# Softmax reciprocals brought to 64 partitions through HBM, and value products in four bursts per pair of heads

## The reference

```python
scores = scale * np.matmul(q, k.transpose(0, 1, 3, 2))
thresh = np.max(scores, axis=-1, keepdims=True) - tau
scores = np.where(scores >= thresh, scores, -1000000000.0)
attn = np.exp(scores - np.max(scores, axis=-1, keepdims=True))
attn = attn / (np.sum(attn, axis=-1, keepdims=True) + 1e-09)
x = np.matmul(attn, v)                      # then (tokens, heads * dim)
h = x @ moe_w_in;  x = (h * np.tanh(softplus(h))) @ moe_w_out
h = x @ moe2_w_in; out = (h * np.clip(h + 3, 0, 6) / 6) @ moe2_w_out
```

## Time and profile before

| | us |
|---|---|
| median of three runs | 1125.66 |
| the profiled execution | 1125.93 |
| its span | 1124.2 |
| PE, busy share of the span | 1108.1 (99%) |
| ACT | 489.7 (44%) |
| DVE | 423.8 (38%) |
| POOL | 263.5 (23%) |

### The profile page before, as it was taken

One profiled execution on the slowest core, in us unless ns is written; L12 is line 12 of the kernel. 1 busy time (PEld: TensorE's weight loads), 2 busy tenths in 40 slices (PEclk: granted clock), 3 DMA queues, 4 the chain that ended last, 5 costly groups with the idle time before them and its releaser, 6 DMA issues.

```text
span 1124.2 us, 15233 instructions
## 1 busy us (share of the span) xinstructions
PE 1108.1 (99%) x6064; PEld 880.3 (78%) x6064; DVE 423.8 (38%) x903; ACT 489.7 (44%) x882; POOL 263.5 (23%) x179
## 2 busy tenths in 40 slices
PE   6999999999999999999999999999999999999998
PEld 5767676767668888889888888888888888888887
DVE  7888787888822111112121111123223223222222
ACT  6777787778744232223222233442232232232232
POOL 6677558655622200000000015420000000000000
PEclk9999999999999999999999999999999999999999
DMA  7432223222021000000000022300010010010010
GB/s 223 127 107 65 84 64 106 64 70 80 12 103 47 1 1 1 1 1 1 1 1 1 19 94 75 112 2 1 1 38 1 1 38 0 1 38 1 1 39 20
DMA packets 42488, 46.09 MB, mean 41 GB/s; under 512 B 3504, under 2 KB 30128, under 8 KB 42416
## 3 DMA queue, kind: packets, MB, share of 16 engines
q1 hardware_dynamic: 42416, 45.10, 13.4%
HBM read 40.37 MB, written 4.72 MB: 40 GB/s over the span
## 4 chain that ended last, share of the span: by engine, by line
PE 97%; DVE 1%; ACT 1%; issue 1%; DMA 0%; SPq 0%; DVEq 0%; ACTq 0%
PE banks L486 35%; PE banks L459 12%; PE banks L461 12%; PE banks L460 12%; PE banks L406 8%; PE banks L353 7%; PE banks L365 5%; PE banks L361 3%; PE banks L386 2%; DVE probs L706 0%; DVE neg_max L722 0%; ACT exps L569 0%; DMA k_raw<-kT 0%; ACT probsT L534 0%; DVE totals L738 0%
## 5 line engine op out<-in xcount | busy, mean ns | idle before, releaser
L767 DVE SCALAR_TENSOR_TENSOR g_low<-gate,g_high 128x512 fp32r<-128x512 f32 (+1 forms) x160 | 102.8, 643 | 478.2 <-ACT g_high L642 478.2
L459 PE MATMUL banks<-x_low,w_in_high 128*128 128x512 f32 (+1 forms) x640 | 239.4, 374 | 0.0
L461 PE MATMUL banks<-x_high,w_in_high 128*128 128x512 f32 (+1 forms) x640 | 238.8, 373 | 0.0
L460 PE MATMUL banks<-x_high,w_in_low 128*128 128x512 f32 (+1 forms) x640 | 237.2, 371 | 0.0
L642 ACT ACTIVATE g_high<-gate 128x512 fp32r<-128x512 f32 (+1 forms) x160 | 94.4, 590 | 310.4 <-PE banks L486 309.9
L459 PEld LDWEIGHTS banks<-x_low,w_in_high 128*128 128x128 f32 x640 | 120.5, 188 | 23.3 <-issue 0.6
L461 PEld LDWEIGHTS banks<-x_high,w_in_high 128*128 128x128 f32 x640 | 120.0, 187 | 23.5
L460 PEld LDWEIGHTS banks<-x_high,w_in_low 128*128 128x128 f32 x640 | 120.7, 189 | 22.4
L722 DVE TENSOR_REDUCE neg_max<-banks 128x1 f32<-128x576 f32 x144 | 108.8, 756 | 50.2 <-PE banks L353 49.9
L486 PE MATMUL banks<-g_low,w_out_high 128*128 128x512 f32 (+1 forms) x320 | 118.3, 370 | 0.8 <-issue 0.8
L486 PE MATMUL banks<-g_high,w_out_low 128*128 128x512 f32 (+1 forms) x320 | 117.8, 368 | 0.0
(11 more groups left out here) (59 smaller groups left out, 1429.8 us busy)
## 6 DMA issues: line engine op xcount, KB each, us to landing
q_raw<-qT SPq DMA_DIRECT2D x64, 144.0 KB, 2.8
k_raw<-kT SPq DMA_DIRECT2D x64, 144.0 KB, 2.8
w_in_raw<-w_in SPq DMA_DIRECT2D x16, 512.0 KB, 4.2
w_out_raw<-w_out SPq DMA_DIRECT2D x16, 512.0 KB, 4.6
out<-x SPq DMA_DIRECT2D x18, 256.0 KB, 2.9
values<-v SPq DMA_DIRECT2D x16, 256.0 KB, 3.1
values<-v SPq DMA_DIRECT2D x16, 32.0 KB, 2.8
tau_in<-tau SPq DMA_DIRECT2D x1, 0.5 KB, 2.8
```

Source lines behind the costliest of these rows:

```text
L459: nc.tensor.matmul(bank, w_in_high[:, t, cols], low, start=(t == 0), stop=False)
L460: nc.tensor.matmul(bank, w_in_low[:, t, cols], high, start=False, stop=False)
L461: mm = nc.tensor.matmul(bank, w_in_high[:, t, cols], high, start=False, stop=(t == KT - 1))
L767: nc.vector.scalar_tensor_tensor(out=g_low[:, f % 2, 0:width], in0=gate[:, f % 2, 0:width], scalar=1 / 6 if layer_of(c) else 1.0, in1=f32( ...
```

## The change

`spread_sums` and ACT's copy of it are dropped. The nine reciprocal columns are instead turned to nine rows by one TensorE transpose in step 2 (`turn_recips`, between the tail transpose and the main ones), into spare columns of a score buffer. ACT copies the rows to SBUF (`keep_recips`), issues a transfer of them to HBM (`store_recips`, 4.6 KB), and in step 4 issues three transfers that read them back, repeated on 64 partitions, to `spread` (`load_spread`). Each head's row lies in one piece or, for the second head, in two. The store waits for the copy, the loads for the store, `scale_mixed` for the loads. Score tile 3, which uses the same buffer, waits for the copy.

The value products of a pair, spread over seven steps before, run in four bursts: part 0 in steps 4 (two key tiles) and 6 (three), part 1 in steps 0 and 1 of the next set (two, three). `scale_mixed` moves from steps 6 and 1 to 8 and 3. In the join the products of each part run in one burst, `turn` is written out, and the wait for `x` stands ahead of the first `down`.

```diff
+    recip_rows = place("recip_rows", [PAIR_TILES, P])
...
+    recip_dram = nc.dram_tensor("recip_dram", (2, PAIR_TILES * P), F32, kind="Internal").ap()
...
+        turned_recips = [banks[0:PAIR_TILES, 2 * s, BANK - P:BANK] for s in range(3)]
...
+        def recip_slot(pair):
+            return 0 if pair < PAIRS - 1 else 2
...
                 if g == EARLY_PIECES:
                     sp.wait_ge(x_ready, 2 * PAIRS)
-                    sp.wait_ge(spread_kept, 2 * PAIRS)
...
+                    if half == 0 and i == 3:
+                        after(pe, recip_rows_kept, t // PAIR_TILES)
...
-            def turn(t, s):
+            def turn_tail(t, s):
                 pe.wait_ge(probs_ready, t + 1)
                 nc.tensor.transpose(turned_tail[s % 3], probs[:, s % 3, SEQ - P:SEQ], ident[:, :]).then_inc(tail_turned, 1)
+            def turn_main(t, s):
                 after(pe, main_kept, t)
                 for j in range(MAIN):
                     mm = nc.tensor.transpose(turned[:, P * j:P * j + P], probs[:, s % 3, P * j:P * j + P], ident[:, :])
                 mm.then_inc(main_turned, 1)
-            def spread_sums(pair, b, u):
-                if u == 0:
-                    pe.wait_ge(recips_ready, pair + 1)
+            def turn_recips(pair, b):
+                pe.wait_ge(recips_ready, pair + 1)
+                nc.tensor.transpose(turned_recips[recip_slot(pair)], recips[:, b, :], ident[:, :]).then_inc(recips_turned, 1)
+            def mix(it, pair, b, u, keys):
+                if keys[0] == 0 and u == 0:
+                    pe.wait_ge(v_loaded[b], 32 * (it + 1 if b == 0 else it))
                     after(pe, x_ready, 2 * pair)
-                else:
-                    pe.wait_ge(spread_kept, 2 * pair + 1)
-                for i in range(MAIN + 1):
-                    c0, c1 = max(P * i, PART_AT[u]), min(P * i + P, PART_AT[u + 1])
-                    for a in range(2):
-                        if c0 < c1:
-                            full = i < MAIN
-                            rows = slice(0, P) if full else slice(TAIL * a, TAIL * a + TAIL)
-                            col = a * (MAIN + 1) + i if full else MAIN
-                            first = 0 if full else TAIL * a
-                            mm = nc.tensor.matmul(mixed[u][DH * a:DH * a + DH, c0 - PART_AT[u]:c1 - PART_AT[u]],
-                                                  recips[rows, b, col:col + 1].to_broadcast([rows.stop - rows.start, DH]),
-                                                  ident[rows, first + c0 - P * i:first + c1 - P * i], start=True, stop=True)
-                mm.then_inc(spread_ready, 1)
-            def mix(it, pair, b, u, keys):
-                if keys[0] == 0 and u == 0:
-                    pe.wait_ge(v_loaded[b], 32 * (it + 1 if b == 0 else it))
-                    pe.wait_ge(spread_kept, 2 * pair + 2)
                     pe.wait_ge(main_kept, (pair + 1) * PAIR_TILES)
                     pe.wait_ge(tail_kept, (pair + 1) * PAIR_TILES)
                 if keys[0] == 0 and u == 1:
@@ -410,8 +407,8 @@
-            part0 = {4: (0,), 5: (1, 2), 6: (3, 4)}
-            part1 = {7: (0, 1), 8: (2,), 0: (3,), 1: (4,)}
+            part0 = {4: (0, 1), 6: (2, 3, 4)}
+            part1 = {0: (0, 1), 1: (2, 3, 4)}
...
             def attention_step(it, s, ahead=True):
@@ -421,16 +418,15 @@
                     score_tile(it, s)
                 pair, b = it * PAIRS_IT + p - 1, (p + 1) % 2
                 if not first or p == 1:
-                    if i in (2, 3):
-                        spread_sums(pair, b, i - 2)
                     if i in part0:
                         mix(it, pair, b, 0, part0[i])
-                    if i in (7, 8):
-                        mix(it, pair, b, 1, part1[i])
-                if not first and i in (0, 1):
+                if not first and i in part1:
                     mix(it, pair - 1, 1 - b, 1, part1[i])
                 if (not first or s >= 2) and (ahead or s < 2):
-                    turn(t - 2, (s - 2) % TILES_IT)
+                    turn_tail(t - 2, (s - 2) % TILES_IT)
+                    if i == 2 and (not first or p == 1):
+                        turn_recips(pair, b)
+                    turn_main(t - 2, (s - 2) % TILES_IT)
...
-            ups_early = {0: 0, 1: 1, 3: 2, 7: 3}
+            UPS_EARLY = 4
...
-            for s in range(PAIR_TILES + 2):
-                if s in ups_early:
-                    pe.wait_ge(tail_kept, ITS * TILES_IT - 2 + ups_early[s] // 2)
-                    up(0, ups_early[s])
-                attention_step(ITS, s, ahead=False)
-            pe.wait_ge(tail_kept, ITS * TILES_IT)
+            def up_early(f):
+                pe.wait_ge(tail_kept, ITS * TILES_IT - 2 + f // 2)
+                up(0, f)
+            last_pair, last_b = PAIRS - 1, PAIRS_IT - 1
+            up_early(0)
+            mix(ITS, last_pair - 1, 1 - last_b, 1, range(MAIN + 1))
+            turn_tail(ITS * TILES_IT - 2, TILES_IT - 2)
+            turn_main(ITS * TILES_IT - 2, TILES_IT - 2)
+            turn_tail(ITS * TILES_IT - 1, TILES_IT - 1)
+            turn_main(ITS * TILES_IT - 1, TILES_IT - 1)
+            turn_recips(last_pair, last_b)
+            up_early(1)
+            up_early(2)
+            mix(ITS, last_pair, last_b, 0, range(MAIN + 1))
+            up_early(3)
+            mix(ITS, last_pair, last_b, 1, range(MAIN + 1))
             pe.wait_ge(main_kept, ITS * TILES_IT)
-            pe.wait_ge(x_ready, 2 * PAIRS)
+            pe.wait_ge(recip_rows_kept, PAIRS)
             for tile in range(STEPS * FT + LAG):
                 c, f = tile // FT, tile % FT
-                if tile < STEPS * FT and not (c == 0 and f in ups_early.values()):
+                if tile < STEPS * FT and not (c == 0 and f < UPS_EARLY):
                     up(c, f)
+                if tile == LAG:
+                    pe.wait_ge(x_ready, 2 * PAIRS)
                 if tile >= LAG:
...
+            def keep_recips(pair):
+                act.wait_ge(recips_turned, pair + 1)
+                after(act, recips_stored, 16 * pair)
+                nc.scalar.copy(recip_rows[:, :], turned_recips[recip_slot(pair)]).then_inc(recip_rows_kept, 1)
+            def store_recips(pair):
+                act.wait_ge(recip_rows_kept, pair + 1)
+                nc.scalar.dma_start(recip_dram[pair % 2].rearrange("(t p) -> t p", p=P), recip_rows[:, :]).then_inc(recips_stored, 16)
+            def load_spread(pair):
+                act.wait_ge(recips_stored, 16 * (pair + 1))
+                after(act, x_ready, 2 * pair)
+                row = recip_dram[pair % 2]
+                nc.scalar.dma_start(spread[0:DH, :], row[0:SEQ].partition_broadcast(DH)).then_inc(spread_loaded, 16)
+                nc.scalar.dma_start(spread[DH:P, 0:MAIN * P], row[SEQ + TAIL:2 * SEQ].partition_broadcast(DH)).then_inc(spread_loaded, 16)
+                nc.scalar.dma_start(spread[DH:P, MAIN * P:SEQ], row[SEQ:SEQ + TAIL].partition_broadcast(DH)).then_inc(spread_loaded, 16)
...
-                if i in (2, 3) and (not first or p == 1):
-                    u, pair = i - 2, it * PAIRS_IT + p - 1
-                    act.wait_ge(spread_ready, 2 * pair + u + 1)
-                    nc.scalar.copy(spread[:, PART_AT[u]:PART_AT[u + 1]], mixed[u]).then_inc(spread_kept, 1)
                 if (not first or s >= 2) and (ahead or s < 2):
                     keep_tail(t - 2, (s - 2) % TILES_IT, it * PAIRS_IT + (s - 2) // PAIR_TILES)
+                if i == 2 and (not first or p == 1):
+                    keep_recips(it * PAIRS_IT + p - 1)
                 if ahead:
                     act.wait_ge(max_ready, t + 1)
                     after(act, probs_ready, t - 1)
                     nc.scalar.activation(halves(exps[:, s % 2, :]), scores[s % 3], ACT.Exp,
                                          bias=neg_max[:, s % 3:s % 3 + 1], scale=1.0).then_inc(exp_ready, 1)
+                if i == 2 and (not first or p == 1):
+                    store_recips(it * PAIRS_IT + p - 1)
+                if i == 4 and (not first or p == 1):
+                    load_spread(it * PAIRS_IT + p - 1)
                 if (not first or s >= 2) and (ahead or s < 2):
                     keep_main(t - 2, (s - 2) % TILES_IT)
...
-                if tile < 2:
-                    attention_step(ITS, tile + 2, ahead=False)
+                if tile == 0:
+                    keep_recips(PAIRS - 1)
+                    store_recips(PAIRS - 1)
+                if tile == 1:
+                    load_spread(PAIRS - 1)
...
+                dve.wait_ge(spread_loaded, 48 * (pair + 1))
...
-                if i == 6 and (not first or p == 1):
+                if i == 8 and (not first or p == 1):
                     scale_mixed(pair, 0)
-                if i == 1 and not first:
+                if i == 3 and not first:
                     scale_mixed(pair - 1, 1)
...
+                    after(dve, recips_turned, pair - 1)
```

(30 more changed lines are left out.)

## The result

The changed kernel takes 1162.51 us, the median of four runs (1157.77 to 1164.14), beside 1125.22 us (1124.62 to 1126.16) for the kernel before on the same chip. The ratio is 1.0323, interval 1.0299 to 1.0346: slower by 37 us. The forecast was 1156, range 1131 to 1175.

What follows compares the result with a forecast made beforehand. PE was taken to bound the kernel, but grouping would expose waits for ACT: 1125.66 + 29.5 (fourteen sets) + 0 (first set) + 0.5 (join) = 1155.7, rounded to 1156 us; range 1131 to 1175.

Steps and rivals of the forecast that it cites:

- The first step, PE's work: Attention loop: dropping L386 and grouping bursts cut PE work by 2.01 us a set, from 19.14 to 17.13.
- the rounding of w_in: ACT, behind step 6 of every second set: delays keep_tail of step 7, costing 0.95 us there, 0.48 a set.
- The waits: Loop steps without a burst: PE waits for ACT's copy, 0.62 us in steps 2, 5, 7, 0.40 in 3, 8.
- PE's 1.29: Loop: PE's time back to its main transposes with no burst between, 0.52 plus 0.61 plus about 0.16 us.
- The issues: ACT's queue, step 4: three loads take 1.62 us, 0.98 exposed in step 5; the store hides behind the exponential.
- Rival (a): Loop: issues cost nothing and travel is hidden, 20.27 us a set, about 1140 in all; chance 0.24.
- The set: One steady set of the loop: 21.25 us in place of 19.14, over fourteen sets +29.5 us.
- The first set: The set before the fourteen full ones, without bursts in steps 0 and 1: 18.56 against 18.54 us, no change.
- The step that failed: Loop transfers: landing 2.8 us after issue, with two or three steps of slack each, hides the travel itself.
- The join: Between loop and layers: the last pair's spread comes over ACT, 23.4 against 22.89 us, +0.5.
- (c): Loop: PE stays the bound because the copies keep up, faster, 1096 us; chance 0.12.
- Rival (d): PE, now with a wait in most steps, is granted a lower clock; chance counted within that of the slower cases.

Runs made afterwards that it cites:

- run four: The kernel before, old reciprocal path kept, with only the value products grouped in four bursts and scale_mixed in steps 8 and 2: 1169.92 us, ratio 1.0393.
- run three: The changed kernel with the seven old bursts and old places of scale_mixed back, reciprocals still through HBM from ACT: 1132.24 us, ratio 1.0058.
- run one: The changed kernel with ACT's load_spread moved from before keep_main of step 4 to behind that of step 5: 1144.73 us, ratio 1.0164.
- run two: The changed kernel with store and loads of all pairs but the last issued by SyncE's queue: 1143.03 us, ratio 1.0151.
- ten: As seven, with SP's eight loads of the first layer's weights issued behind the first pair's transfers: 1129.55 us, ratio 1.0035.
- run twelve: As run eleven, with ACT's first rounding of the weights moved from ahead of the second iteration to its seventh step: 1121.74 us, ratio 0.9953.
- run nine: The changed kernel with only the first pair's three loads issued later, in step 5 behind keep_main: 1159.16 us, ratio 1.0286.
- run five: The changed kernel with seven old bursts back and transfers of all pairs but the last on SyncE: 1128.55 us, ratio 1.002.
- seven: The changed kernel with seven old bursts, transfers of all pairs but the last on SyncE, and keep_main ahead of the exponential: 1126.52 us, ratio 1.0006.
- run eleven: As ten, with GpSimd rounding, from the second iteration on, the two keys that ACT rounded: 1123.09 us, ratio 0.9977.

## Why the prediction was right

**The first step, PE's work.** Forecast 19.14 - 2.01 = 17.13 a set. Over the span PE's busy time fell by 13.1, only 0.8 a set, and a set shows 18.02 or 18.25 busy. Most of the difference is the way stops are booked. A tail transpose followed at once takes 0.17 up to the next start (187.34 to 187.51), a lone one ahead of a wait 0.27; the main transposes take 0.36 to the next start in a row and 0.41 after a wait. So a stop books 0.15 of itself as busy time, and five or six stops a set (steps 2, 3, 5, 7, 8, and one more with the rounding of w_in) make 0.75 to 0.9. In step 2 the wait of the score tile for `keep_recips` is booked the same way: its start comes 0.65 after that of the main transposes, not 0.41. What can be checked by itself came as said: the burst of three key tiles at 256 columns, 0.22 + 3 x 0.43 + 0.15 = 1.66, is in the trace with 1.66 (PE in a late set):

```profile
340.03 1.66 PE L403 MATMUL banks<-probsT,values 128*64 128x256 f32 x12
```

**The waits.** Right in kind and place. Forecast 0.62 in steps 2, 5 and 7 and 0.40 in 3 and 8, from the chain of keep_tail, exponential and keep_main against PE's 1.29. The profile books less, 0.52 in step 7, 0.41 in step 2, 0.23 or 0.60 in step 8 and none in step 3, but from start to start step 7 is as forecast:

```profile
194.14 0.27 PE L374 MATMUL banks<-ident,probs 128*128 128x128 f32 x1
194.93 0.66 PE L380 MATMUL banks<-ident,probs 128*128 128x128 f32 x4 [0.52 <-ACT probsT L543]
```

These are 0.79 apart where an unhindered pair is 0.17 apart, so 0.62 are lost. Step 2 comes to 0.62 in the same way; steps 3 and 8 come to 0.24 and 0.33, less than the 0.40. So the total is right mostly because its terms are, and not because PE's work and the waits happened to be off by the same amount. The direct proof that the missing cover does it is run four, where nothing but the bursts (and their scale) was changed, and run three, where they are back and the wait falls from 47.3 to 10.5 us. One reading of the trace before was wrong and did no harm: not "every step but two or three" but all nine of a set held a burst or a reciprocal product.

**The issues.** Forecast 0.98 exposed, in step 5, behind an exponential that hides the store and 0.64 of the loads. Measured 0.91; the store cost nothing beside the exponential in the steady state. Runs one and two confirm the price (0.9 a set). Rival (a), that the issues cost nothing, is refuted by the row at 189.65. The Trainium skill's page named in the prediction ("Perfetto Trace Analysis", DMA Instruction — HWDGE, and DVE / Act Engine Instruction) gave about the same 0.9, and the trace agrees: the first load is issued 0.15 us into `keep_tail`, while the engine still has that copy and the exponential to run.

**The set.** Forecast 21.25, measured 20.86 and 21.77 in turn, mean 21.3: 2.19 more a set than before, where 2.11 was forecast. That two kinds alternate is the rounding of w_in in every second set, forecast as 0.95 and seen as 0.91 between these two.

**The first set, the term that was mis-sized.** The prediction gave ±0; it measured +5.85, nearly all of the distance between 1156 and 1162.5. The step that failed is the one by which a landing 2.8 us after the issue, with two or three steps of slack, "hides the travel itself". I had not asked what else was in flight when the first store went out. ACT and PE in the changed kernel:

```profile
29.72 0.66 ACTq L571 DMA_DIRECT2D recip_dram<-recip_rows  x1
36.28 0.50 ACTq L578 DMA_DIRECT2D spread<-recip_dram  x1
...
38.10 0.58 ACT L543 COPY probsT<-banks 128x512 f32<-128x512 f32 x1 [3.00 <-issue]
```

```profile
38.74 1.12 PE L380 MATMUL banks<-ident,probs 128*128 128x128 f32 x4 [3.63 <-ACT probsT L543]
...
40.75 3.02 PE L403 MATMUL banks<-probsT,values 128*64 128x256 f32 x12
```

The store is issued at 29.72, but the loads, which wait for it in ACT's queue, go out only at 36.28. SP had issued eight weight loads of 512 KB from 16.4 to 24.6 us and eight issues of heads behind them; the window 28.83:54.21 moves 142 GB/s. The exponential ended at 35.1, the copy then stood 3.00 us, PE 3.63. After that PE's granted clock is 0.50 (1.2 GHz) from 38.7 to 44.0, and the burst that takes 1.66 takes 3.02; PE's 5.26 us of busy time there would be half at full clock, so by my estimate about 3 us of the 5.85 are the stand and 2.6 the clock. Run one removes the whole loss by taking the waiting issue out from ahead of the copy. That it was the weights in flight that held the store back is shown by runs ten and twelve, where they come behind it: there the first load follows the first store after 1.28 and 1.27 us (29.60 to 30.88, 29.54 to 30.81). The Trainium skill ("TensorE: Matmul & The Clock Gate", What's actually happening) says that the clock is gated by how busy PE has been recently; the rows of the first set agree, while run nine's two falls can't be told from the busy time in its rows.

**The join.** Forecast +0.5, measured +0.12. ACT stood 3.94 us for the last pair's store as well, but its `scale_mixed` ran at 365.05 and PE lost only 0.37 us to it (L403 at 365.56).

**The rivals.** (c), PE stays the bound, is false as the change stands; PE comes nearest to it with old bursts, transfers off ACT, the copy first and keys on GpSimd (18.45 a set, where (c) had 17.1). Rival (d), a lower granted clock, came true in a part that I hadn't priced, and not by its reason. It named PE's waits in most steps, but from 54.21 to the end of the loop, where these waits are, the clock is 1.00; in the profiled run nearly all of the fall is in the first set, behind the one long stop. Over the four runs the time goes roughly with the clock (1157.77 at 1.000, 1161.64 at 0.997, 1163.38 at 0.993, 1164.14 at 0.994), so it may be worth up to some 6 us; where the clock fell in the runs that weren't profiled isn't known.

**What stays open.** That sets alternate in runs five, seven and ten is ACT's rounding of keys, since run eleven moves only that and makes them even; by which wait it costs PE its microsecond wasn't followed. What makes the clock fall in run nine without a long wait isn't known: sets with the same busy time ran at full clock. One set of run two did the same (22.35 us at 0.92). That run twelve's second set can be mended by placing the second pair's store ahead of the query load was not tried.

## What to carry to other kernels

Small pieces of work of the bound engine between its dependent steps are cover: before they are grouped to save their openings, write out the chain through the other engines and see which steps are left bare; here 0.5 us of openings a set bought about 2 us of waits for the copy (30.4 us over 15 sets in run one), and 0.9 more for the issues. A transfer that waits for another transfer belongs behind what the next engine needs, or in a queue where nothing is urgent, and its landing is to be judged by what is in flight at that moment, the first time round above all. After a repair look at the queue that was given the work: three times here (five, ten, twelve) the same loss came back one place on.

## What was unexpected of the hardware

- A 4.6 KB store whose dependents go out about 1.2 us later in the steady state (in run five, store at 207.49, first load at 208.71) took 6.56 us (29.72 to 36.28) with the weight loads and heads in flight.
- ACT's queue issued a transfer 0.15 us after the start of the copy two instructions ahead of it, and the issue of a ready store ran wholly beside the exponential; issuing the nine rows took 0.27 us in the steady state and 0.66 in the first set, a load repeated on 64 partitions 0.45 to 0.62.
- The granted clock fell to its lower level after one wait of 3.63 us, and stayed at 1.00 through the first set of run three with a wait of 2.70 at the same place. In run nine it averaged 0.66 and 0.81 over some microseconds with no wait for the copy over 1.6 us ahead, while four other sets of the same kind ran at 1.00.
